# Products of 40 rows read as 64, and a full product ahead of each join of solved blocks

## What is computed

```python
# batch 4, heads 8, steps 768, head size D = 40
for t in range(S):
    y[:, :, t] = einsum('bhd,bhde->bhe', r_t, state)
    Sa = einsum('bhde,bhe->bhd', state, a_t)
    state = state * w_t[:, :, None, :] - einsum('bhd,bhe->bhde', Sa, b_t) \
            + einsum('bhd,bhe->bhde', v_t, k_t)
x = y as [3072 tokens, 320]
# first mixture: x @ w_gate -> argmax expert e, softmax weight g, sigmoid output gate
out[tok] = g * sigmoid(x @ w_output_gate)[e] * (relu(x @ w1[e]) @ w2[e])
# second mixture: the same without the output gate, capacity 768 tokens an expert
```

## Time and profile before

| | |
|---|---|
| median of 3 runs | 1418.29 us (1409.77 to 1421.76) |
| profiled execution | 1407.96 us, its span 1406.2 us |
| mean granted clock of TensorE | 0.822 |
| PE busy | 1096.3 us, 78% |
| PE weight loads | 936.2 us, 67% |
| DVE, ACT, POOL busy | 485.9, 288.2, 376.1 us |

### The profile page before, as it was taken

One profiled execution on the slowest core, in us unless ns is written; L12 is line 12 of the kernel. 1 busy time (PEld: TensorE's weight loads), 2 busy tenths in 40 slices (PEclk: granted clock), 3 DMA queues, 4 the chain that ended last, 5 costly groups with the idle time before them and its releaser, 6 DMA issues.

```text
span 1406.2 us, 45504 instructions
## 1 busy us (share of the span) xinstructions
PE 1096.3 (78%) x19760; PEld 936.2 (67%) x19761; DVE 485.9 (35%) x867; ACT 288.2 (20%) x548; POOL 376.1 (27%) x350
## 2 busy tenths in 40 slices
PE   1278677777888788882399999999540999998996
PEld 0268677767877677740288888888310888886884
DVE  5653356434543443024023223322150233232321
ACT  0133334343443334420011011011100110110010
POOL 4233234332443142103412222212016122121211
PEclk8556777677576767796599999999875999999998
DMA  2234344443444322051214225240503033335000
GB/s 82 65 89 118 87 106 111 113 118 77 112 123 113 84 61 54 13 150 38 89 34 143 86 89 155 87 150 23 187 8 114 29 110 108 106 109 175 32 28 1
DMA packets 158724, 125.76 MB, mean 89 GB/s; under 512 B 91498, under 2 KB 136046, under 8 KB 158576
## 3 DMA queue, kind: packets, MB, share of 16 engines
q1 hardware_dynamic: 139216, 93.53, 23.9%
q10 hardware_dynamic: 12096, 14.09, 3.4%
q0 software_dynamic: 7264, 15.86, 3.2%
HBM read 89.57 MB, written 36.16 MB: 89 GB/s over the span
## 4 chain that ended last, share of the span: by engine, by line
PE 57%; DVE 13%; DMA 10%; SPq 8%; issue 5%; POOL 4%; ACT 1%; POOLq 0%; DVEq 0%; ACTq 0%
PE pair L1179 18%; PE pair L1160 16%; DVE products L1252 6%; PE pair L1167 5%; POOL x_sorted L603 3%; SPq L414 3%; DVE T_rows L1257 3%; SPq L395 3%; PE pair L1122 2%; PE pair L1147 2%; DMA G_rows<-g_dram 2%; DMA g_dram<-G_b 2%; DMA tn_dram<-T_nat 2%; PE pair L882 2%; DMA D_nat<-tn_dram 1%
## 5 line engine op out<-in xcount | busy, mean ns | idle before, releaser
L1179 PE MATMUL pair<-abk_in,H_nat 128*128 x992 | 278.6, 434 | 1.7 <-DVE y_T L1431 1.7
L1160 PEld LDWEIGHTS pair<-y_T,rvm 128*128 128x128 f32 x1984 | 237.5, 197 | 19.2 <-issue 6.8
L1160 PE MATMUL pair<-y_T,rvm 128*128 128x128 f32 x1984 | 238.7, 280 | 8.2 <-DVE rvm L1416 5.8
L1179 PEld LDWEIGHTS pair<-abk_in,H_nat 128*128 128x128 f32 x992 | 184.0, 190 | 71.7 <-issue 2.7
L795 ACT ACTIVATE H_nat<-pair 128x512 f32<-128x512 f32 x62 | 37.0, 597 | 525.3 <-PE pair L1167 525.3
L1416 DVE COPY rvm<-AG 128x2560 f32 x62 | 95.2, 1536 | 99.4 <-issue 79.4
L1252 DVE TENSOR_TENSOR products<-T_rows,G_rows 128x1 f32<-128x1 f32 (+4 forms) x180 | 96.1, 534 | 69.3 <-DMA G_rows<-g_dram 63.5
L1147 PE MATMUL pair<-table_sb,y_T 128*128 128x128 f32 x186 | 34.6, 296 | 92.5 <-DMA y_T<-x_sorted 92.5
L556 POOL TENSOR_SCALAR_AFFINE_SELECT rvm<-rvm 64x1024 f32<-64x1024 f32 x48 | 54.9, 1143 | 151.8 <-ACT rvm L644 150.1
L1423 DVE TENSOR_SCALAR H_nat<-pair 128x512 f32<-128x512 f32 x62 | 42.8, 690 | 144.3 <-PE pair L1167 144.2
L556 POOL TENSOR_SCALAR_AFFINE_SELECT AG<-AG 64x512 f32<-64x512 f32 x48 | 31.4, 654 | 219.9 <-ACT AG L644 217.5
(11 more groups left out here) (141 smaller groups left out, 1587.6 us busy)
## 6 DMA issues: line engine op xcount, KB each, us to landing
abk_in<-w SPq DMA_DIRECT2D x16, 1280.0 KB, 8.3
y_T<-x_sorted ACTq DMA_DIRECT2D x62, 160.0 KB, 2.2
AG<-w SPq DMA_DIRECT2D x16, 512.0 KB, 3.5
AG<-w SPq DMA_DIRECT2D x32, 256.0 KB, 4.4
x_sorted<-empty SPq DMA_DIRECT2D x6, 1288.0 KB, 7.3
t_dram<-T_rows SPq DMA_DIRECT2D x12, 384.0 KB, 2.3
AG<-w SPq DMA_DIRECT2D x32, 128.0 KB, 4.8
w_in<-wT SPq DMA_DIRECT2D x48, 80.0 KB
```

What stands on the lines that cost most here:

```text
L1160: mm(to, w1_now[:, par, k * F + m * P:k * F + m * P + P], xT[:, (0, 2 - m // 4)[k], :], start=(m % 4 == 0 and k == 0), stop=False, skip_gr ...
L1179: last = mm(bank[5][:, 0:DM], hidT[par][:, k, :], ring2[:, bass.ds(place, 1), k, :].rearrange("p a d -> p (a d)"), start=(k == 0), stop=(k ...
```

## The change

Six products that contract over the 40 elements of a head read 64 partitions instead, the 24 more being those that were cleared at the start: in `grams_b`, `grams_k`, `natural`, `state_natural` and both of `inner`. Second, a new function `full_rows(b)` makes one product with the 128 x 128 identity and the first 256 columns of the constant table over the full array, into a bank that the stage behind it overwrites. It is called once in each of `join_first`, `join_second`, `quotient` and `corner`, after their waits and before their products, so 4 times a set and 48 times in all. Nothing reads its result.

```diff
--- before.py
+++ after.py
@@ -818,6 +818,10 @@
         def _(pe):
             mm = nc.tensor.matmul
 
+            def full_rows(b):
+                mm(b[:, 0:256], ident, table_sb[:, 0:256], start=True, stop=True)
+
+
             def grams_b(k):
                 pe.wait_ge(b_scaled, k + 1)
                 pe.wait_ge(a_scaled, 4 * (k + 1))
@@ -827,8 +831,8 @@
                     for a in range(NPAIR):
                         for b, o in WAYS:
                             last = mm(pair[1][half_rows(b ^ o), o, c * 256 + a * C:c * 256 + (a + 1) * C],
-                                      AG[head_rows(o), (2 * k + c) % 5, o, b, a, :],
-                                      b_in[k % 2][head_rows(o), b, a, c * C:(c + 1) * C], start=True, stop=True)
+                                      AG[half_rows(o), (2 * k + c) % 5, o, b, a, :],
+                                      b_in[k % 2][half_rows(o), b, a, c * C:(c + 1) * C], start=True, stop=True)
                 last.then_inc(gb_ready, 1)
 
             def grams_k(u):
@@ -846,8 +850,8 @@
                         at = (b * NPAIR + a) * C
                         for o in range(2):
                             last = mm(pair[1][half_rows(1 - o), o, at:at + C],
-                                      k_in[k % 2][head_rows(o), b, a, c * C:(c + 1) * C],
-                                      AG[head_rows(o), u % 5, o, b, a, :], start=True, stop=True)
+                                      k_in[k % 2][half_rows(o), b, a, c * C:(c + 1) * C],
+                                      AG[half_rows(o), u % 5, o, b, a, :], start=True, stop=True)
                 last.then_inc(gk_ready, 1)
 
             def natural(u):
@@ -863,8 +867,8 @@
                         for other, t in enumerate((b_in[k % 2], k_in[k % 2])):
                             for o in range(2):
                                 last = mm(pair[2][half_rows(o ^ other), o, at:at + D],
-                                          t[head_rows(o), b, a, c * C:(c + 1) * C],
-                                          eyes[head_rows(o)], start=True, stop=True)
+                                          t[half_rows(o), b, a, c * C:(c + 1) * C],
+                                          eyes[half_rows(o)], start=True, stop=True)
                 last.then_inc(nat_ready, 1)
 
             def join_first(k):
@@ -872,6 +876,7 @@
                 if k + 1 < NK:
                     pe.wait_ge(gb_copied, k + 2)
                 pe.wait_ge(gk_copied, 2 * (2 * k + 1))
+                full_rows(pair[1][:, 0, :])
                 for m in range(2):
                     for c in range(CC):
                         for a in range(NPAIR):
@@ -888,6 +893,7 @@
             def join_second(k):
                 pe.wait_ge(ga_copied, 2 * (k + 1))
                 pe.wait_ge(nat_copied, 2 * k + 2)
+                full_rows(pair[2][:, 0, :])
                 for m in range(2):
                     for x in range(CC * H):
                         for h in range(2):
@@ -952,8 +960,8 @@
                     for a in range(NPAIR):
                         at = (b * NPAIR + a) * D
                         for o in range(2):
-                            q = head_rows(o)
-                            last = mm(pair[0][q, o, at:at + D], ZV[q, u % 4, o, b, a, :], eyes[q],
+                            q, rows = head_rows(o), half_rows(o)
+                            last = mm(pair[0][q, o, at:at + D], ZV[rows, u % 4, o, b, a, :], eyes[rows],
                                       start=True, stop=True)
                 last.then_inc(sn_ready, 1)
 
@@ -1008,11 +1016,11 @@
                         at = (b * NPAIR + a) * C
                         rt = slice(c * C, (c + 1) * C)
                         for o in range(2):
-                            q = head_rows(o)
+                            q = half_rows(o)
                             mm(pair[2][half_rows(o), o, at:at + C], U_T[q, b ^ o, a, :], r_in[k % 2][q, b, a, rt],
                                start=True, stop=True)
                         for o in range(2):
-                            q = head_rows(o)
+                            q = half_rows(o)
                             last = mm(pair[2][half_rows(1 - o), o, at:at + C], vT_in[k % 2][q, b, a, rt],
                                       r_in[k % 2][q, b, a, rt], start=True, stop=True)
                 last.then_inc(m_ready, 1)
```

## The result

| | before | changed |
|---|---|---|
| median of 20 runs | 1416.18 us | 1422.94 us |
| lowest to highest | 1409.77 to 1421.76 | 1414.41 to 1431.10 |
| profiled execution | 1407.96 us, span 1406.2 | 1426.46 us, span 1424.8 |
| its mean granted clock | 0.822 | 0.844 |

The ratio is 1.0051, with a 95% interval of 1.0035 to 1.0068: 0.5% slower, 6.8 us between the medians. I had predicted +8 us over the median shown. So the traces are read for where and how, and the medians for how much.

What follows compares the result with a forecast made beforehand. In most recurrence rounds queues, DMA and the DVE solve bound the kernel, PE only from join to k products. Terms 8 + 3 + 2 + 9 - 6.5 - 7.5 = +8 us on 1418.29 gave 1426, range 1399 to 1448.

Steps and rivals of the forecast that it cites:

- The chain: Recurrence rounds: G and T through DRAM and the solve set the pace; PE counts only from join to k products.
- Rows cost nothing: Six lines reading 64 partitions in place of 40: taken as 0, at most 6 ns of an overlapped latency.
- The price of a pair: One full product's two records: 0.6 us at 2.4 GHz, 1.05 at 1.2, with the next stage behind, not beside.
- join_first: Its full product, behind the wait for T, on the chain in nine rounds at 0.9 us: +8 (5 to 9.5).
- The other three in a waiting round: Full products of join_second, quotient and corner: 2.7 us against 2.5 idle, some rounds running over: +3 (0 to 8).
- join_second's delay of POOL: Its product delays inner, masks and POOL's scaling by 0.3 us against the solve, in nine rounds: +2 (-6 to +7).
- Rounds without a wait: Round from 387 us and last two sets: 12 full products +9 (7 to 12.6), higher clock -7.5 (0 to -15).
- The clock: More rows ahead of a stage lift its level: -6.5 on the chain in waiting rounds, -7.5 in rounds without a wait.
- the rest: Rounds without a wait, +9, with the clock's gains of -6.5 in waiting rounds and -7.5 in the others.
- the rival, a lifted clock: Rival for the follow-up with join_first's product alone: lifting the join's clock gives part back, ratio 1.003 or less; no chance stated.

Runs made afterwards that it cites:

- the row of four pairs: Four full products in the idle time ahead of join_first's wait for T, with the 64 rows and those of quotient and corner; 0.9994 to the kernel before.

## Why the prediction was right, and where its terms were not

Right in sign and size (+8 against +6.8), and in what carries it: a full product on the chain behind the wait that ends last. Step by step:

- *The chain* held: a round is set by G's and T's way through DRAM and the solve, and PE's place in it is the join to the k products. Solves stayed as they were, 13.7 us before and 13.6 after as the mean of the second to tenth round.
- *Rows cost nothing*: shown, by `inner`'s 0.37 us with 40 and with 64 rows, and by the kernel with the rows alone, -1 us.
- *The price of a pair*, 0.6 and 1.05 us worked out from the earlier trace rows, was a little small: a pair takes 0.70 us at the high level and 1.22 at the low one (0.98 in the chain above, where the clock was 0.65 over the pair), and the stage behind starts 0.07 us before its modelled end. So it costs 0.63 or 1.15, and 0.5 in the row of four pairs in 1.99 us. The record itself was worked out at 379 ns and is 379. That the next stage starts behind the pair, and not beside it, held.
- *join_first*, +8 (5 to 9.5): mis-sized. It measures 13 us in the changed kernel and about 3 beside the rows alone. For the changed kernel the trace has the reason: all twelve joins wait, not nine, and seven of the twelve pairs ran at 1.15 us, one at 0.91 and four at 0.63. That makes 11.5 us.
- *The other three in a waiting round*, +3, and *join_second's delay of POOL*, +2: together the wrong sign. Beside the rows they bring 5 us, give or take 4 (0.9957 against 0.9994), and don't cost 5. The cover was larger than the 2.5 us that I set against 2.7: the kernel with the rows alone waits 29.1 us in ten joins, 2.9 each.
- *Rounds without a wait*, +9 and -7.5 of clock: there are none now, all twelve joins wait. From the eleventh join to the last full transpose of `turn_y` the kernel before takes 87.3 us and the changed one 88.1.
- *The clock*, -14 in all: it rose over the execution, but not where it was to pay. In the piece on the chain the mean clock is 0.65 before and 0.60 after, and its length 8.5 and 8.9 us, in the same nine rounds. The 0.65 owes much to the one round without a wait, at 387 us, whose piece ran at 1.00; now every round waits. A higher level would pay there: over these nine pieces in each of eleven traces, the time in which PE works in a piece is 8.0 us on average where its clock is 0.50 to 0.55 (37 pieces) and 5.6 where it is 1.00 (4). The difference of 2.2 us between the two pieces in the earlier trace rows, which I put down mostly to the clock, is mostly gaps: 2.50 us in the long piece and 0.89 in the short one, 1.6 of the 2.2, at mean clocks of 0.62 and 0.70. That was the misreading: a difference between two pieces of a chain was given to the clock before its pieces were looked at. The full products do cost 11 us less with the rows than without (1.0130 to 1.0051, give or take 6). In the two traces the 48 pairs take 46.3 us with the rows and 49.9 without; where the rest of it comes from isn't shown.

So terms that were too small and too large on one side met terms of the other kind: +13 for `join_first` against 8, -5 against +5 for the other three, about 0 for the rest against -5. The sum is right partly by chance.

**Open.** Why `join_first`'s product costs 13 us beside the other three and about 3 without them. The 13 are the full price, as the 11.5 us of the trace show; what has to be explained is the 3. In the two traces of the kernel with this product alone it delays the twelve joins by 10.4 and 9.5 us, so something gives some 7 back. PE's piece behind it is shorter there (8.4 and 8.6 us against 9.1 and 8.8 with the rows alone), which is the way of the rival, a lifted clock; but two executions of the kernel without this product differ by as much (9.1 and 8.6). The runs don't separate them. Nor is it shown in a trace where the 5 us of the other three come from: the profiled executions of those kernels, at 1412 to 1414 us of span, were among the slowest of theirs. In the two profiled executions compared above, the rounds of the changed kernel are 1.6 us longer: 0.4 in PE's piece, 0.2 from there to the solve, and 1.2 from the solve's end to the join, 0.9 of it the full product itself.

## What to carry to other kernels

Ask of every filler product which wait stands behind it: in this kernel the same 256 columns cost 13 us behind the wait that ends last (with the other three in place), some 5 or less ahead of it, and nothing where the engine has slack. A higher granted clock is worth only what the pieces on the chain become shorter; here it rose from 0.81 to 0.85 over an execution and much of it became idle time before the next join. And before a difference between two rounds is put down to the clock, list what is in them: a gap in which nothing is issued looks the same in a sum.

## What the runs showed of the hardware

- Reading 64 rows in place of 40, with zeros in the 24, raised the mean granted clock of an execution from 0.812 to 0.835 at the same number of instructions. Full-array products of 256 columns alone left it at 0.812; the two together gave 0.846. I had expected a part from each. (The Trainium skill, "TensorE: Matmul & The Clock Gate", Part 1, says the gate goes by how busy PE has been. The runs don't bear out that busy time alone decides: PE was busy 12.69 of 12.70 us at 0.50, and from before to the kernel with the rows alone the clock in the windows above rose from 0.72 to 0.74 while PE's busy time fell from 452.6 to 437.5 us. A higher clock shortens the busy time by itself, so this fall is no cause; but the rows added no busy time either.)
- The join's tiles of 32 rows and 16 columns take 1.69 us for 128 records at a clock of 1.00 and 1.82 at 0.50 (the joins at 339.93 and 293.39 in the earlier trace rows), so the clock has little hold on them. The k products, of 64 columns, take 1.10 and 1.91 us.
- PE has gaps inside a stage, with no wait that the profile shows, of up to 2.9 us before the change (160.48) and 4.4 after it (496.90). They come at steps of 127 or so matmul records, at the same places of the program with and without the change.
